# Three-stage attention and mixture kernel: the last, 64-row tile of each expert of the second mixture takes its high and low parts in one pass, and a search round takes two exchanges instead of three

## The reference

```python
cap = N // E                      # 4608 // 8 = 576
order = np.argsort(-flat)         # all (row, expert) logits, largest first
for idx in order:
    tok, e = (int(idx) // E, int(idx) % E)
    if assigned[tok] >= 0 or counts[e] >= cap:
        continue
    assigned[tok] = e
    counts[e] += 1
...
    h = np.maximum(x[mask] @ w1[e], 0.0)
    out[mask] = h @ w2[e]
```

## Time and profile before

| what | value |
|---|---|
| median of 3 runs | 1489.16 us (1486.3 to 1492.13) |
| the profiled execution's own time | 1488.37 us |
| its span, first to last instruction | 1486.6 us |
| mean granted TensorE clock | 0.941 of full |
| busy: TensorE / VectorE / ScalarE / GpSimd | 89% / 63% / 30% / 27% |
| chain that ended last: TensorE / VectorE / DMA / issue | 67% / 12% / 7% / 6% |

### The profile page before, as it was taken

One profiled execution on the slowest core, in us unless ns is written; L12 is line 12 of the kernel. 1 busy time (PEld: TensorE's weight loads), 2 busy tenths in 40 slices (PEclk: granted clock), 3 DMA queues, 4 the chain that ended last, 5 costly groups with the idle time before them and its releaser, 6 DMA issues.

```text
span 1486.6 us, 23689 instructions
## 1 busy us (share of the span) xinstructions
PE 1317.2 (89%) x8032; PEld 1053.5 (71%) x8032; DVE 939.4 (63%) x2238; ACT 444.3 (30%) x785; POOL 398.9 (27%) x323
## 2 busy tenths in 40 slices
PE   5988717897999999999995279999999999999997
PEld 5877616786888888888884156777677677777885
DVE  1566794677577776776676757676566656675520
ACT  1555521222222222222220112323232223323431
POOL 1244425757515271570000010202020111111210
PEclk9899958999999999999997579999999999999999
DMA  9999127695415153351100313131313131413100
GB/s 230 259 236 308 57 53 283 213 358 176 143 44 156 44 157 93 107 156 44 44 29 15 113 36 121 54 128 50 132 44 138 45 139 36 146 36 138 51 32 18
DMA packets 71155, 173.27 MB, mean 117 GB/s; under 512 B 11624, under 2 KB 30136, under 8 KB 70400
## 3 DMA queue, kind: packets, MB, share of 16 engines
q1 hardware_dynamic: 46576, 108.61, 24.0%
q0 software_dynamic: 12368, 40.92, 8.8%
q10 hardware_dynamic: 12096, 22.19, 4.7%
HBM read 130.47 MB, written 41.23 MB: 115 GB/s over the span
## 4 chain that ended last, share of the span: by engine, by line
PE 67%; DVE 12%; DMA 7%; issue 6%; POOL 6%; ACT 1%; SPq 1%; POOLq 0%; DVEq 0%; ACTq 0%
PE bank L719 52%; PE bank L762 4%; POOL w_lo L557 3%; DMA xst<-x_rows,tok_i 2%; PE bank L818 2%; PE o_ps L681 2%; PE bank L755 2%; DVE cmp L1298 1%; DMA x_sorted<-xst 1%; DMA v_sb<-in_v 1%; POOL xrow L565 1%; DVE ohb L1388 1%; DMA w_sb<-in_moe_w 1%; POOL w_hi L555 1%; PE bank L748 1%
## 5 line engine op out<-in xcount | busy, mean ns | idle before, releaser
L1280 DVE SCALAR_TENSOR_TENSOR bank<-bank,factor,wg2b 128x512 f32<-128x512 f32 x336 | 254.6, 758 | 10.4
L1267 DVE TENSOR_TENSOR hT_lo<-bank,hT_hi 128x512 fp32r<-128x512 f32 x166 | 106.7, 684 | 184.9 <-ACT hT_hi L1008 184.8
L719 PE MATMUL bank<-w_hi,xT_hi 128*128 (+1 forms) x664 | 199.2, 417 | 12.5 <-POOL w_lo L557 7.7
L975 ACT ACTIVATE h<-bank 128x512 f32<-128x512 f32 x166 | 99.3, 598 | 356.7 <-PE bank L719 356.7
L719 PE MATMUL bank<-w_lo,xT_hi 128*128 (+1 forms) x664 | 192.7, 407 | 0.0
L611 POOL DMA_INDIRECT xg<-y_rows,gat_i x40 | 45.6, 1140 | 545.2 <-DVE sca_i L1398 400.5
L719 PE MATMUL bank<-w_hi,xT_lo 128*128 (+1 forms) x664 | 187.6, 403 | 0.0
L719 PE MATMUL bank<-w_hi,hT_hi 128*128 (+1 forms) x664 | 180.8, 412 | 6.2 <-DVE score L1283 3.9
L719 PE MATMUL bank<-w_hi,hT_lo 128*128 (+1 forms) x664 | 175.7, 400 | 0.0
L719 PE MATMUL bank<-w_lo,hT_hi 128*128 (+1 forms) x664 | 173.6, 399 | 0.0
L719 PEld LDWEIGHTS bank<-w_hi,xT_lo 128*128 128x128 f32 x664 | 125.8, 191 | 30.0
(11 more groups left out here) (243 smaller groups left out, 1677.5 us busy)
## 6 DMA issues: line engine op xcount, KB each, us to landing
w_sb<-in_moe_w SPq DMA_DIRECT2D x112, 512.0 KB, 6.3
y_rows<-y ACTq DMA_DIRECT2D x43, 256.0 KB, 3.0
x_sorted<-xst SPq DMA_DIRECT2D x41, 260.0 KB, 5.6
xg<-x_sorted ACTq DMA_DIRECT2D x41, 260.0 KB, 2.8
k_sb<-in_k SPq DMA_DIRECT2D x16, 576.0 KB, 12.0
v_sb<-in_v SPq DMA_DIRECT2D x16, 576.0 KB, 14.9
q_sb<-in_q SPq DMA_DIRECT2D x8, 1152.0 KB, 17.7
x_rows<-xrow POOLq DMA_DIRECT2D x16, 576.0 KB, 6.7
```

Of the source, the lines that this page charges most:

```text
L719: mm = pe.matmul(ps, a[:, i % chunks, :], b[:, i % chunks, cols], start=(i == 0), stop=(i == 3 * chunks - 1))
L975: act.activation(h[:, half * HALF:(half + 1) * HALF], h_ps[half][:, :], ACT.Relu).then_inc(s_h, 1)
L1267: dve.tensor_tensor(hT_lo[:, half * 4:(half + 1) * 4, :].rearrange("p a b -> p (a b)"), th_ps[half][:, :], hT_hi[:, half * 4:(half + 1) * ...
L1280: ch.link(dve.scalar_tensor_tensor(out=prod_ps[:, :], in0=y1_ps[t % 2][:, :], scalar=factor[:, t:t + 1], in1=wg2b[:, e, :], op0=ALU.mult, ...
```

## The change

Two things change in the second mixture.

**The last tile of an expert** (64 rows) keeps its high part in stationary columns 0 to 63 and its low part in columns 64 to 127 of the same tile. One pass with the high weights gives both products (rows 0 to 63 and 64 to 127 of the result), and a second pass with the low weights uses only the 64 high columns. So there are 2 x chunks matmuls instead of 3 x chunks. The halves of h are added while they are turned: the transposes of that tile become real fp32 matmuls with a 128 x 64 matrix `fold` of two identities, and the ReLU moves behind them. The halves of y are added by a ScalarE copy (`upper_y`) and a VectorE addition (`halves_added`). The short tile's first and second layer have 8 slots each instead of 12, and an expert 112 slots.

**A search round** has two exchanges. VectorE itself picks the diagonal blocks (a multiplication and a sum), adds the room and spreads the result by expert; one TensorE matmul of 120 columns spreads it over the partitions. The places of the exchanges and of the work beside them are written anew. ScalarE makes all eight high weight pieces of the next expert in the last three tiles (3, 3, 2).

```diff
-    PER_TILE = 24
-    cycle = PER_TILE * T2
-    RANKS_BEHIND, LIST_BEHIND, LISTED = 3, 9, 10
+    FULL, SHORT = 6, 4
+    for g in range(T2):
+        FIRST_AT.append(cycle)
+        cycle += 2 * (SHORT if g == T2 - 1 else FULL)
+        SECOND_AT.append(cycle)
+        cycle += 2 * (SHORT if g == 0 else FULL)
+    RANKS_BEHIND, LIST_BEHIND, LISTED = 2, 6, 7
...
-    WHERE = timed(-64, (10, 11, 15, 11, 11, 11, 11, 11), 3, (0, 3, 8, 13))
-    FIRST = [None] * (LISTED + 1) + [1] + timed(6, (8, 8, 8, 8), 3, (1, 4, 9, 13))
+    WHERE = timed(-63, ((10, 3), (11, 3), (16, 7), (10, 3), (9, 3), (9, 3), (10, 3), (10, 3)), (0, 3, 8, 14))
+    FIRST = [None] * (LISTED + 1) + timed(1, ((8, 3),) * 4, (0, 3, 8, 12))
...
-    LOW_BESIDE = {11: (0,), 12: (1,), 13: (2,), 14: (3,), 19: (4,), 20: (5,), 22: (6,), 23: (7,)}
+    LOW_BESIDE = {8: (0,), 9: (1,), 10: (2,), 11: (3,), 13: (4,), 14: (5,), 15: (6,), 16: (7,)}
...
+            def short_in_parts(ps, act, w, cols, chunks, high_w, low_w, low_x, done, point):
+                pe.wait_ge(*low_x)
...
+                order = [(0, P), *((c, LAST) for c in range(chunks)), *((c, P) for c in range(1, chunks))]
+                for i, (c, rows) in enumerate(order):
+                    mm = pe.matmul(ps[0:rows, :], act[:, c, 0:rows], w[rows < P][:, c, cols],
+                                   start=(i == 0), stop=(i == 2 * chunks - 1))
...
+                        if short:
+                            mm = pe.matmul(th_ps[half][:, i * P:i * P + LAST], h[:, half * 4 + i:F:FC], fold[:, :], start=True, stop=True)
+                            continue
...
-                    pe.matmul(cps[0:E, 0:NTH], room_n[:, :], ones_h[0:1, 0:NTH], start=True, stop=False)
-                    for g in range(GROUP):
-                        mm = pe.matmul(cps[0:E, 0:NTH], ident_h[:, g * E:(g + 1) * E], dense[:, g * NTH:(g + 1) * NTH],
-                                       start=False, stop=(g == GROUP - 1))
-                elif n < 3 * R:
-                    mm = pe.matmul(aps[:, 0:NTH], ones_h[0:E, :], ind[:, :], start=True, stop=True)
+                    mm = pe.matmul(cps[:, 0:E * NTH], ones_h[0:GROUP * E, :], dense[:, :, :].rearrange("p e n -> p (e n)"),
+                                   start=True, stop=True)
...
+            def upper_y(j, u):
...
+                act.activation(upper, y_ps[LAST:2 * LAST, :], ACT.Copy).then_inc(s_yu, 1)
...
+            def halves_added(kk, u):
...
+                dve.wait_ge(s_yu, kk + 1)
...
+                dve.tensor_tensor(ys[w % 2][0:LAST, :], y_ps[0:LAST, :], upper, ALU.add).then_inc(s_y, 1)
...
-                ch.inc(dve.tensor_scalar(room_n[:, :], room[0:1, :], -1.0, None, ALU.mult))
+                link(dve.tensor_tensor(room8[:, :], room[0:GROUP * E, :], less_own[:, :], ALU.mult))
+                ch.inc(dve.tensor_reduce(room_n[:, :], room8[:, :], AX, ALU.add))
...
-                    ask(dve.tensor_copy(dense[:, :], dps[0:GROUP * E, :]))
-                    ask(dve.tensor_scalar(ind[:, :], cps[0:E, 0:NTH], 0.0, None, ALU.is_ge))
-                    link(dve.scalar_tensor_tensor(out=tn[:, :], in0=aps[:, 0:NTH], scalar=0.5, in1=weights[:, r, :],
-                                                  op0=ALU.is_gt, op1=ALU.mult))
-                    link(dve.tensor_reduce(n_i[:, r:r + 1], tn[:, :], AX, ALU.max))
+                    link(dve.tensor_tensor(counts[:, :, :], dps[0:GROUP * E, :].rearrange("p (g n) -> p g n", n=NTH),
+                                           own_group[:, :].unsqueeze(2).to_broadcast([GROUP * E, GROUP, NTH]), ALU.mult))
+                    link(dve.tensor_reduce(count[:, :], counts[:, :, :].rearrange("p g n -> p n g"), AX, ALU.add))
+                    ask(dve.scalar_tensor_tensor(out=dense[:, :, :], in0=count[:, :].unsqueeze(1).to_broadcast([GROUP * E, E, NTH]),
+                                                 scalar=room_n[:, 0:1], in1=own_expert[:, :].unsqueeze(2).to_broadcast([GROUP * E, E, NTH]),
+                                                 op0=ALU.add, op1=ALU.mult))
+                    link(dve.scalar_tensor_tensor(out=tn[:, :, :], in0=cps[:, 0:E * NTH].rearrange("p (e n) -> p e n", n=NTH), scalar=0.0,
+                                                  in1=weights[:, r, :].unsqueeze(1).to_broadcast([P, E, NTH]), op0=ALU.is_ge, op1=ALU.mult))
+                    link(dve.tensor_reduce(n_i[:, r:r + 1], tn[:, :, :].rearrange("p e n -> p (e n)"), AX, ALU.max))
```

More of the change, by code:

```diff
@@ L85, in build, with timed @@
     GROUP = 4
-    SUMS, TOTALS, TIES = range(3 * R, 3 * R + 3)
-    STEPS = 3 * R + 3
+    SUMS, TOTALS, TIES = range(2 * R, 2 * R + 3)
+    STEPS = 2 * R + 3
     BIDS = STEPS
-    PER_TILE = 24
-    cycle = PER_TILE * T2
-    RANKS_BEHIND, LIST_BEHIND, LISTED = 3, 9, 10
-    def timed(start, rounds, spread, behind):
+    FULL, SHORT = 6, 4
+    FIRST_AT, SECOND_AT, cycle = [], [], 0
+    for g in range(T2):
[4 more added lines that the diff above has]
+    RANKS_BEHIND, LIST_BEHIND, LISTED = 2, 6, 7
+    def timed(start, rounds, behind):
         at = []
-        for gap in rounds:
-            at += [start + spread * i for i in range(3)]
+        for gap, spread in rounds:
+            at += [start, start + spread]
             start += gap
@@ L388, in build @@
         sc1 = sb("sc1", [P, 8])
-        ind = sb("ind", [E, NTH], F16)
-        dense = sb("dense", [GROUP * E, GROUP * NTH], F16)
+        counts = sb("counts", [GROUP * E, GROUP, NTH])
+        count = sb("count", [GROUP * E, NTH])
+        dense = sb("dense", [GROUP * E, E, NTH], F16)
         owner = sb("owner", [P, T1])
@@ L753, in y_rows_in, with h_turned @@
                 pe.wait_ge(s_yg[w % 2], (j * T2 + (w // 2 + 1)) * 16)
+                rows = LAST if vv == T2 - 1 else P
+                if rows < P:
+                    alone(pe)
                 for c in range(KC):
-                    mm = pe.transpose(tx_ps[:, c * P:(c + 1) * P], xgs[w % 2][:, c:DM:KC], ident[:, :])
+                    mm = pe.transpose(tx_ps[:, c * P:c * P + rows], xgs[w % 2][0:rows, c:DM:KC], ident[0:rows, 0:rows])
                 mm.then_inc(s_tx, 1)
-            def h_turned(n):
+            def h_turned(n, short=False):
                 for half in range(2):
@@ L813, in search @@
                     alone(pe)
[L814 removed]
+                if n < 2 * R and n % 2 == 0:
                     for g in range(0, T1, GROUP):
@@ L884, in phase @@
                     n = kk * T2 + (T1 + vv)
+                    short = vv == T2 - 1
                     if vv == 0:
@@ L887, in phase @@
                     low = kk * PIECES + PIECES // 2 if vv == 0 else None
-                    first_in_parts(n, w1_parts, 0, low, lambda i: searches(kk, PER_TILE * vv + i))
-                    first_in_parts(n, w1_parts, 1, None, lambda i: searches(kk, PER_TILE * vv + 6 + i))
+                    for half in range(2):
+                        at = FIRST_AT[vv] + half * (SHORT if short else FULL)
+                        first_in_parts(n, w1_parts, half, low if half == 0 else None, lambda i: searches(kk, at + i), short)
                     if vv < T2 - 1 or not fixed or kk < E - 1:
@@ L894, in phase @@
                         second_in_parts(n - 1, w2_before if vv == 0 else w2_parts, all_w, all_w,
-                                        lambda i: searches(kk, PER_TILE * vv + 12 + i))
+                                        lambda i: searches(kk, SECOND_AT[vv] + i), vv == 0)
                     else:
-                        for i in range(PER_TILE // 2):
-                            searches(kk, PER_TILE * vv + 12 + i)
-                    h_turned(n)
+                        for i in range(2 * SHORT):
+                            searches(kk, SECOND_AT[vv] + i)
+                    h_turned(n, short)
             for n in range(STEPS):
@@ L912, in _ @@
             phase(E // 2 - 1, 1)
-            second_in_parts(NT2 + T1 - 1, [split_w[2 + i][1] for i in range(2)], None, None, lambda i: None)
+            second_in_parts(NT2 + T1 - 1, [split_w[2 + i][1] for i in range(2)], None, None, lambda i: None, True)
         @block.scalar
@@ L1350, in duties @@
                     if kind == "h" and not (fixed and tile == 0):
-                        hT_low(T1 + tile - 1)
+                        hT_low(T1 + tile - 1, g == 0)
                     elif kind == "x" and not (fixed and tile == NT2 - 1):
-                        rows_low(T1 + tile + 1)
+                        rows_low(T1 + tile + 1, g == T2 - 2)
+                    elif kind == "y" and not (fixed and tile == 0):
+                        halves_added(kk - 1, 1 - u)
             tied, rank, chosen, mine, cum = (m43[:, i, :] for i in (0, 2, 3, 4, 5))
```

135 lines of the change are left out of this document (92 added, 43 removed).

## The result

The changed kernel takes 1468.78 us (median of four runs, 1468.52 to 1471.91), the kernel before 1490.64 beside it. The ratio is 0.9872, with a 95% interval of 0.9849 to 0.9894: 1.3% faster, some 20 us. Forecast were 35 us less and 1454, in a range from 1442 to 1469; little more than half of the gain came. The time lies at the upper edge of the range, and the ratio applied to the 1489.16 us that the forecast started from gives 1470, just outside. The profiled execution took 1468.89 us, its span is 1467.1.

A forecast was written before the change was run, and what follows sets the result against it. The prediction took TensorE's queue, its own work and its waits for VectorE, as the bound. Its terms (-29.9 + 6.5 - 19.0 - 2.4 + 4.9 - 2.0 + 5.0 + 1.4) gave -35.5 against 1488.4, rounded to 1454 us; range 1442 to 1469.

The forecast's parts named there:

- Short tiles: Second mixture, last tile of each of eight experts: 16 of 48 matmuls go, 29.9 us saved on TensorE's path.
- The fold: Turning of the short tile's h: 8 fp32 matmuls as 16 records of 0.10 us, 6.5 us added, between nothing and 19.
- Exchanges: Search rounds beside the experts: each loses the 0.40 us diagonal exchange, its spreading matmul costs 0.04 more; 19.0 us saved together.
- small stalls: TensorE's waits for one-hots in an expert shrink, one of about 0.5 us at TIES remains; 2.4 us gained over six experts.
- VectorE's load: VectorE's busy time in an expert rises from 50.9 to about 55.5 us of some 71, and fits if never late.
- rival (a): VectorE late in several search rounds, half of the exchanges missing by 0.3 us: 18 us lost, 1472 us; chance 0.14.
- rival (c): VectorE's handshake is the bound, its idle time does not shrink, and the kernel becomes slower: 1517 us; chance 0.03.
- Loop ends: Where VectorE goes round its loop: fewer slots and a longer chain make TensorE wait longer; 4.9 us lost, phase 0 included.
- Phase 0: 12 slots without matmuls, where TensorE served exchanges at VectorE's pace, become 8 with one full comparison bare: 2.0 us gained.
- The search alone: Search rounds where TensorE has nothing else: 0.34 us more a round in the first search; 5.0 us added in all.
- The tail: End of the program: last short second layer waits for h's low half, last y gets copy and addition; 1.4 us added.
- Rival (b): The fold takes four records or does not overlap: 13 us more, 1467 us; chance 0.05.

## Why the prediction was right and wrong

*Short tiles, -29.9*: the matmuls are as counted; a short tile's 16 of one layer, 8 of them with 64 stationary columns, take 3.72 us on the chain, 0.233 each.

*The fold, +6.5*: this is the step that failed. The forecast said "the record is set by the load of its 128 stationary columns, as for the transposes: 0.10 us". The count of records and the limit by the load were right. But the price came from L803, whose columns lie side by side, and from transposes, and the fold's columns lie 8 elements apart. The record measured 0.227 us, the fold cost 2.8 us more than transposes, 22.6 in all, 16 more than the term. The run with transposes in its place, 25 us faster, shows that this is what was missing. The high end of that term, 19 us, would have given 1466. By its own condition it was too low: two records of 0.256 us without overlap, less the 0.10 of a transpose, are 0.41 us a matmul, 26 us in all, and 1474. So a range that held the whole of the term would have reached over what was measured. The Trainium skill's four passes (FP8 and Floating Point Precision, TensorE Precision Notes) gave nearly this sum, though by a mechanism that the runs do not show: there are two records, and with adjacent columns they cost 0.106 us each.

*Exchanges, -19.0; small stalls, -2.4*: right and slightly too careful. 2.9 + 0.4 were forecast for an expert, and 4.0 came (76.58 - 71.68 = 4.90, of which 3.74 - 2.83 = 0.9 are the short tile's). The wait of 0.5 at TIES did not come; TensorE has none in the windows without a loop end.

*VectorE's load*: 55.5 us forecast, 55.9 measured, and TensorE does not wait for it away from the loop end, so neither rival (a) nor rival (c) came. With 68.9 us an expert it still kept up.

*Loop ends, 3.6 of the +4.9*: the difference between the two kinds of expert grew from 4.2 and 5.7 us to 6.8 and 6.9, by 2.6 and 1.2. The mean of 1.9 is the 1.8 forecast, but that is luck. The 5.7 us before hold a wait of TensorE for a high weight piece, which no term of the forecast was about and which the kernel after does not have:

```profile
1183.28 0.73 PE L719 MATMUL bank<-w_hi,xT_hi 128*128 128x512 f32 x2 [1.78 <-ACT w_hi L1015]
```

Without it a loop end grew by 2.6 and 3.0 us, 2.0 more than forecast for the two: the wait of 4.05 us is longer than the 3.3 forecast (the forecast's own 1.2 on top of 2.47 would have made 3.7), and the low clock behind it lasts 6 us instead of 3, which the forecast left as it was. In four of the runs above (transposes, adjacent columns with and without the loop, the search alone) the wait is there again, 1.5 to 1.8 us; why the kernel after has none, the runs do not settle.

*Phase 0, -2.0*: the waits for VectorE in the slots without matmuls fell from 4.1 us (1.68, 0.30, 0.41 and 1.67) to 2.3 (0.29 and 2.04), 1.7 gained. The 1.3 us of the loop's term that were meant for this phase came out at 0.8 (waits of 0.55 and 2.15 became 2.77 and 0.77).

*The search alone, +5.0*: from the end of the first mixture to the first rows of the second lie 864.12 - 794.00 = 70.12 us, and 859.97 - 795.40 = 64.57 before, so +5.6.

*The tail, +1.4*: too small. From the start of the last turning to the end of the span it was 16.9 us and is 20.9. With 2.8 more for the fold and 1.9 less for eight matmuls, 3.0 are left: 1.3 for copy and addition (from the start of y's copy to its scatter it was 0.87 us and is 2.22), the rest the low clock in the last 16 matmuls and a little waiting.

*Left out of the forecast*: the granted clock falls behind the fold without any wait in two experts, 1.3 and 1.6 us. So the sum had no term for what the fold does to the matmuls behind it.

The sum with the measured terms: 35.5 - 16.1 (fold) - 1.6 (tail) - 2.9 (clock) - 0.6 (search alone) - 2.0 (loop ends) + 0.2 (phase 0) makes 12.5, and 0.7 us more from exchanges and stalls in each of six experts, 4.2, makes 16.7. The wait for a high weight piece that is gone adds 1.8 and the stages ahead of the search, which the change does not touch, 1.4. That makes 19.9; 19.5 lie between the two profiled executions. Rival (b), the fold dearer than its records say, is the one that came true in its size, and its cause was not among the two that it named. It had a chance of 0.05.

## What to carry to other kernels

A matrix product with a small constant matrix is not as cheap as a transpose: here a real fp32 matmul loads its stationary side twice (128 loads for 64 matmuls), and its records are 2.1 times as far apart if the columns lie 8 elements apart (0.227 against 0.106 us). Look up the price of an operation in a row with the same stride, type and mode, and if only two of these agree, keep the upper bound as a case with weight. Where TensorE is the bound and VectorE has 15 us of slack in 71, an addition of two halves belongs on VectorE. Before two profiled executions are subtracted, look whether the stages that are the same in both took the same time.

## What the runs showed of the hardware

In a real fp32 matmul the load of 128 stationary columns that lie 8 elements apart takes 335 ns, against 192 for adjacent ones and 190 for a transpose's with the same spacing; the number of moving columns, 64 or 8, changes nothing in it. At the branch back of its loop VectorE issues nothing for 5.55 us before and 6.15 after, and in the trace with the loop written out there is no such hole. TensorE's granted clock can fall from 2.4 to 1.2 GHz right behind 3.6 us of the strided loads, during which TensorE never waited; from trace to trace it did so behind none, two or six of seven folds.
